# Order changes around a product scheme: second-layer operands, two plain projections, weight sums

## The reference

```
scores = scale * q @ k.T          # 4 x 8 heads of 576 x 64
ret    = scores * Dmat            # Dmat[i, j] = gamma_h ** (i - j) for i >= j, else 0
x      = (ret @ v), heads side by side                       # 2304 x 512
h      = x @ w_in                                            # 2304 x 2048
g      = h if h >= 1; 0 if h <= -1; (h + 1)**2 / 4 between   # the gate
x      = g @ w_out                                           # 2304 x 512
out    = ((x @ w_a) * (x @ w_b)) @ w_out2                    # 2304 x 1536, then 2304 x 512
```

## Time and profile before

| | |
|---|---|
| median of the runs | 897.81 us |
| profiled execution, its own time | 899.2 us |
| span in its profile | 897.4 us |
| PE busy | 864.2 us, 96% |
| DVE busy | 516.6 us, 58% |
| ACT busy | 349.0 us, 39% |
| POOL busy | 186.7 us, 21% |

### The profile page before, as it was taken

How to read it: one execution, slowest core, us unless ns; L and a number is a source line. 1 busy time by engine, 2 the same in 40 slices (tenths; PEclk the granted TensorE clock), 3 DMA queues, 4 the chain that set the end, 5 groups by cost and what they waited for, 6 DMA issues and landing times.

```text
span 897.4 us, 14103 instructions
## 1 busy us (share of the span) xinstructions
PE 864.2 (96%) x5520; PEld 825.6 (92%) x5520; DVE 516.6 (58%) x873; ACT 349.0 (39%) x650; POOL 186.7 (21%) x198
## 2 busy tenths in 40 slices
PE   7999999999999999999899888999999999999998
PEld 6989998999899999999899877889999999999996
DVE  4686777674545764446866555674434475434353
ACT  1235664554553443434433444342223242223220
POOL 4652125301422232323452233100000000000000
PEclk9999999999999999999999999999999999999999
DMA  9999179867453644463253744565454755454622
GB/s 354 322 367 360 45 248 379 334 218 294 173 184 125 249 176 168 173 237 139 106 203 161 280 190 159 215 235 211 165 211 164 247 199 211 165 211 164 209 73 70
DMA packets 47665, 188.35 MB, mean 210 GB/s; under 512 B 3568, under 2 KB 16368, under 8 KB 38896
## 3 DMA queue, kind: packets, MB, share of 16 engines
q1 hardware_dynamic: 47456, 187.26, 56.9%
q10 hardware_dynamic: 144, 0.20, 0.1%
HBM read 137.63 MB, written 49.81 MB: 209 GB/s over the span
## 4 chain that ended last, share of the span: by engine, by line
PE 80%; DVE 11%; ACT 4%; issue 2%; DMA 1%; SPq 1%; POOL 0%; ACTq 0%; DVEq 0%; POOLq 0%
PE score_b L684 7%; PE score_b L688 7%; PE score_b L686 7%; PE score_a L684 5%; PE score_a L688 5%; PE score_a L686 5%; PE kv_b L724 3%; PE kv_b L725 3%; PE kv_b L723 3%; PE ret_b L724 3%; PE ret_b L725 3%; PE ret_b L723 3%; PE ret_b L707 2%; PE ret_b L705 2%; PE kv_b L707 2%; PE kv_b L705 2%
## 5 line engine op out<-in xcount | busy, mean ns | idle before, releaser
L684 PE MATMUL score_b<-xop_hi,wop 128*128 128x384 f32 x416 | 140.3, 337 | 10.5 <-DVE wop L843 7.3
L688 PE MATMUL score_b<-xop_hi,wop 128*128 128x384 f32 x416 | 139.5, 335 | 0.0
L686 PE MATMUL score_b<-xop_lo,wop 128*128 128x384 f32 x416 | 139.3, 335 | 0.0
L684 PE MATMUL score_a<-xop_hi,wop 128*128 128x384 f32 x312 | 104.7, 336 | 9.1 <-DVE wop L843 6.0
L686 PE MATMUL score_a<-xop_lo,wop 128*128 128x384 f32 x312 | 104.2, 334 | 0.0
L688 PE MATMUL score_a<-xop_hi,wop 128*128 128x384 f32 x312 | 104.2, 334 | 0.0
L684 PEld LDWEIGHTS score_b<-xop_hi,wop 128*128 128x128 f32 x416 | 78.1, 188 | 14.8 <-issue 8.8
L686 PEld LDWEIGHTS score_b<-xop_lo,wop 128*128 128x128 f32 x416 | 78.1, 188 | 1.2
L688 PEld LDWEIGHTS score_b<-xop_hi,wop 128*128 128x128 f32 x416 | 78.1, 188 | 0.0
L1230 ACT ACTIVATE p<-score_b 128x384 f32<-128x384 f32 x52 | 25.5, 490 | 115.7 <-PE score_b L688 115.7
L684 PEld LDWEIGHTS score_a<-xop_hi,wop 128*128 128x128 f32 x312 | 58.6, 188 | 10.8 <-issue 10.2
(11 more groups left out here) (166 smaller groups left out, 2120.2 us busy)
## 6 DMA issues: line engine op xcount, KB each, us to landing
wop<-w_ops SPq DMA_DIRECT2D x40, 1792.0 KB, 7.3
w_ops<-wop SPq DMA_DIRECT2D x12, 1792.0 KB, 6.0
kq<-k_q SPq DMA_DIRECT2D x16, 576.0 KB, 6.8
wo_raw<-w_out SPq DMA_DIRECT2D x9, 1024.0 KB, 9.8
kvt<-kv_tok SPq DMA_DIRECT2D x16, 512.0 KB, 5.8
w_ops<-s_op SPq DMA_DIRECT2D x8, 1024.0 KB, 5.9
wo_hi<-w_outs SPq DMA_DIRECT2D x8, 1024.0 KB, 6.9
wo_lo<-w_outs SPq DMA_DIRECT2D x8, 1024.0 KB, 9.1
```

Source lines behind the costliest of these rows:

```text
L684: pe.matmul(o, w[:, 0, at], xop_hi[b][:, k, :], start=(start and k == 0), stop=False, skip_group_check=True)
L686: pe.matmul(o, w[:, 0, at], xop_lo[b][:, k, :], start=False, stop=False, skip_group_check=True)
L688: mm = pe.matmul(o, w[:, 1, at], xop_hi[b][:, k, :], start=False, stop=(k == 1), skip_group_check=True)
```

## The change

- **Second layer's operands.** The sums' half of step u + 1 is rounded and split in the middle of step u (before: at its end), and the raw half of step u + 2 at the end of step u (before: that of u + 1 in its middle). POOL does all four low parts of a step first, and then the sums of u + 2 instead of u + 1.
- **Last two projections.** `project(1, 14)` moves from ahead of the product steps into step 0, and `project(1, 15)` from step 0 into step 1, both before product 5. `copy_y` of tile 1 moves from step 1 to step 2.
- **Copies and gate.** In steps 0 to 2 ACT copies product 5 right after the third relu. The gate's four relus write prod0, prod1, prod0, prod1 instead of prod1, prod0, prod0, prod1; the first waits for DVE's gate and no longer for POOL.
- **Weights' sums.** The table of gates behind which the eight sets are rounded and split changes, and SP issues the load and the slabs of pair p + 2 ahead of the store of set p.

```diff
-        prep_steps = {(0, 10): 0, (0, 12): 1, (0, 14): 2, (1, 0): 3, (1, 2): 4, (1, 4): 5, (1, 6): 6,
+        prep_steps = {(0, 9): 0, (0, 12): 1, (1, 1): 2, (1, 2): 3, (1, 4): 4, (1, 5): 5, (1, 7): 6,
                       (1, 8): 7}
...
+            for p in range(2):
+                load_s(p)
+            for p in range(2):
+                store_slabs(p)
             for p in range(NF1 // 2):
-                load_s(p)
-                store_slabs(p)
-                if p:
-                    store_s(p - 1)
-            store_s(NF1 // 2 - 1)
+                if p + 2 < NF1 // 2:
+                    load_s(p + 2)
+                    store_slabs(p + 2)
+                store_s(p)
...
                 if v <= V1:
-                    low_parts(v - 1, 0)
-                    low_parts(v - 1, 1)
-                if 0 <= v + 1 - V1 < NF2:
-                    second_sums(v + 1 - V1)
-                if v <= V1:
-                    low_parts(v - 1, 2)
-                    low_parts(v - 1, 3)
+                    for i in range(4):
+                        low_parts(v - 1, i)
+                if 0 <= v + 2 - V1 < NF2:
+                    second_sums(v + 2 - V1)
...
-            project(NT - 1, NF1 - 2)
...
-                if v == 0:
-                    project(NT - 1, NF1 - 1)
-                else:
+                if v:
                     pe.wait_ge(u2_copied, v)
                     product(7, v - 1, main_b[(v - 1) % 2], False).then_inc(p7_done, 1)
+                if v < 2:
+                    project(NT - 1, NF1 - 2 + v)
...
-                s = [prod1, prod0, prod0, prod1][i]
+                s = [prod0, prod1, prod0, prod1][i]
...
-                if v == 1:
+                if v == 2:
                     copy_y(NT - 1)
                 if 0 <= u + 1 < NF2:
-                    split_ops(u + 1, 0)
+                    split_ops(u + 1, 1)
...
-                if 0 <= u + 1 < NF2:
-                    split_ops(u + 1, 1)
+                if 0 <= u + 2 < NF2:
+                    split_ops(u + 2, 0)
...
-                if p and i < 2:
+                if p and i == 0:
+                    act.wait_ge(g_ready, 4 * p - 1)
+                elif p and i == 1:
                     act.wait_ge(gl1_ready, 4 * p)
                 elif i >= 2:
-                    act.wait_ge(g_ready, 4 * p + 2)
-                    if i == 3:
-                        act.wait_ge(gl1_ready, 4 * p)
+                    act.wait_ge(g_ready, 4 * p + i - 1)
...
-                if 0 <= u + 1 < NF2:
-                    round_ops(u + 1, 0)
                 if gated_before:
                     gate_relu(v - 1, 2)
+                if v < 3:
+                    copy_p5(v)
+                if gated_before:
                     gate_high(v - 1, 2)
...
+                if 0 <= u + 1 < NF2:
+                    round_ops(u + 1, 1)
-                if v == 1:
+                if v == 2:
                     copy_y(NT - 1)
...
-                if v < V:
-                    if v:
-                        act.wait_ge(b1_ready, v)
-                    act.wait_ge(p5_done, v + 1)
-                    nc.scalar.activation(p5[:, :], p5_b, ACT.Copy).then_inc(p5_copied, 1)
+                if 3 <= v < V:
+                    copy_p5(v)
...
-                if 0 <= u + 1 < NF2:
-                    round_ops(u + 1, 1)
+                if 0 <= u + 2 < NF2:
+                    round_ops(u + 2, 0)
```

More of the change, by code:

```diff
@@ L1186, in gate_high, with copy_p5 @@
                                      ACT.Copy).then_inc(gh1_ready, 1)
+            def copy_p5(v):
+                if v:
+                    act.wait_ge(b1_ready, v)
+                act.wait_ge(p5_done, v + 1)
+                nc.scalar.activation(p5[:, :], p5_b, ACT.Copy).then_inc(p5_copied, 1)
             def step(v):
```

## The result

The changed kernel takes 890.82 us (median of 4 runs, 889.48 to 892.33), before 897.78 (4 runs). The ratio is 0.992, 95% interval 0.9908 to 0.9933. It is faster by 7.0 us, where 18.8 were forecast; 890.8 lies above the range of 874 to 886. The profiled execution took 892.33 us, span 890.5.

A forecast was written before the change was run, and what follows sets the result against it. PE bounds the kernel, its matmuls unchanged, so only its idle or slow time can shrink. Gains of 14.2 + 2.0 + 2.6 = 18.8 us gave 879.0 us; forecast 876 to 882, range 874 to 886.

The forecast's parts named there:

- Term 1: Second layer's steps: operands written half a step sooner remove PE's waits on wop, net gain 14.2 us (10.5 to 16.0).
- ten waits: PE's waits for DVE's wop write before the second layer's steps 0, 1, 4 to 11: 16.0 us, all to go.
- what comes back: Second layer's steps 3 and 4: other work limits them, so 0.9 us each, 1.8 us, of the gain is lost.
- The second rival: Second layer: DVE replaces wop as the bound, half of eight waits returns, time 886 us; chance 0.13.
- Term 2: Plain tiles and weights' sums: gain at the change of tiles less a tile 1 wait, net 2.0 us (-3 to 5.2).
- The gain at the change of tiles: Change of plain tiles: xl starts sooner and partly escapes POOL's sums, gaining 3.0 us (1.5 to 5.2).
- The first rival: Tile 1: the weights' sums become the wait, making term 2 -3 us and the time 884; chance 0.15.
- set 7: Tile 1: POOL's last set of the weights' sums was to begin at 175.5 and end at 179.5.
- the gap: Tile 1, ahead of the projection of f = 9: PE waits some 1.0 us for gl.
- The turn from a set to the next but one: Weights' sums in tile 1: 6.2 us of SP issues, 5.9 of landing and 4.3 of sums, 16.4 us.
- they now stand ahead of each store of sums: Tile 1: SP's load and four slab stores, 6.2 us, precede each store of sums and make the sums later.
- Term 3: First product steps: last two projections in steps 0 and 1 cover ACT and DVE, gaining 2.6 us (1.5 to 3.45).

The follow-up runs named there:

- 12: Changed kernel with fourth wop load first, slabs early, POOL waiting for xl, later y copies; plus sums' half split behind prod0 in steps 3, 4: 877.97 us.
- 11: Changed kernel with fourth wop load first, slabs early, POOL waiting for xl, later y copies; plus three POOL sums in each of steps 3, 4: 878.85 us.
- 8: Changed kernel with the fourth wop load first and the table of gates as before, SP's order still new: 882.62 us.
- 7: Changed kernel with the fourth wop load first and SP's order as before, the table of gates still new: 885.83 us.
- 6: Changed kernel with the fourth wop load first, all slabs stored during tile 0 and six sets of sums one gate sooner: 880.44 us.
- experiment 3: Changed kernel with the fourth product step's wop load issued ahead of the first two output weights' loads: 884.66 us.

## Why the prediction was wrong

**Term 1 held in its mechanism and was 1.2 us too large.** All ten waits went, as said. The term was 14.2 and is 13.0; what I mis-sized was what comes back. By PE's starts of product 1 the second layer's steps 3 and 4 took 17.8 us before (487.43 to the 505.25 of the earlier trace rows) and take 17.5 now:

```profile
487.43 0.33 PE L684 MATMUL score_b<-xop_hi,wop 128*128 128x384 f32 x1
```

```profile
491.28 0.33 PE L682 MATMUL score_b<-xop_hi,wop 128*128 128x384 f32 x1
...
499.22 0.45 PE L682 MATMUL score_a<-xop_hi,wop 128*128 128x384 f32 x1
...
508.74 0.44 PE L682 MATMUL score_b<-xop_hi,wop 128*128 128x384 f32 x1
```

Waits of 2.9 us have gone from them and they are only 0.4 us shorter, so 2.5 us came back there instead of 1.8. Another 1.5 came back in step 0, where I had put nothing: the wait of 1.05 us ahead of step 1 went, but PE now waits 1.2 us for b in the step, which got 0.5 us longer. The later steps gave 1.0 us more than their waits. What step 4 of the changed kernel spends its time on can be read from ACT and DVE:

```profile
505.40 0.53 ACT L1226 ACTIVATE ph<-prod 128x384 fp32r<-128x384 f32 x1 [1.87 <-DVE prod L978]
505.83 1.04 ACT L1063 ACTIVATE wop<-wop_sum 128x1024 fp32r<-128x1024 f32 x1
```

```profile
506.91 1.31 DVE L841 TENSOR_TENSOR wop<-wop_sum,wop 128x1024 fp32r<-128x1024 f32 x1 [1.60 <-ACT wop L1063]
508.14 0.55 DVE L992 TENSOR_TENSOR prod<-score_b,a 128x384 f32<-128x384 f32 x1
```

ACT rounds prod1's product (505.40) and then the sums' half (505.83); DVE waits 1.60 us for this, splits it (506.91), and only then multiplies prod0 (508.14). Prod0 ends at 508.69, and product 1 of step 5, which needs it, starts at 508.74. So the two engines take turns, and I had summed each engine's work, not the turns. This chain is read from the trace. Taking the split out of it (12) shortened the two steps by only 0.5 us, because product 1 needs the split too; so that the turns and no other limit set these steps is argued, not shown. POOL's part in it is small (11). The second rival was right in kind for these two steps, but not for the long ones.

**Term 2: the gain was larger and the loss much larger.** The gain at the change of tiles is 4.3 us (3.0 forecast). The first rival came: POOL's set 7 began 3.4 us later than estimated, and I had given the gap 1.0 us. It was 4.25 us (4.4 from matmul to matmul), and I had no price for what follows a gap of that length: nearly 5 us of matmuls at the lower level of 1.2 GHz, which lost 2.3 us more. PE was also 0.5 us later than before when it came to the change of tiles, for which no part of the change accounts. 4.3 - 4.4 - 2.3 - 0.5 is the net of -2.7 that the marks show, to within 0.2. The rival's -3 had that size, and I gave it 0.15. The turn from a set to the next but one, 16.4 us in the estimate, was 17.4 and 18.6, with landings of 7.2 to 8.2 us where I took 5.9; and my own sum for set 7 slipped by 0.5 us, since 159.6 + 16.4 is 176.0 and not 175.5. The step as I put it ("they now stand ahead of each store of sums") blamed SP's order, which is nearly free (8); the new table of gates makes the chain late (7), and slabs stored in tile 1 seem to keep it late (6, where gates and slabs were moved together).

**Term 3 failed, and it took the forecast out of its range.** The step was "the last two projections ... stand in steps 0 and 1 and cover what ACT and DVE do there". They did, and saved 4.2 us by the marks, or 2.8 by experiment 3, where 2.6 were forecast. But I asked only ACT and DVE who is helped by the later end of a projection, not SP, which waits for exactly that end ahead of the output weights' loads; and behind these in one queue stands the load that step 3 needs. The wait and the low clock after it, 7.6 us by the marks, are the largest part of the 11.9 us missing; with one load moved ahead in SP's order (3) 6.2 of them came back, to 884.66 us, inside the range. Had I priced only this and kept the rest, the forecast would have been 886.6, and with the measured term 2 in its place 891.3; the errors of term 1 and of what term 3 saves nearly cancel.

## What to carry to other kernels

When work is moved on the engine that sets the time, list everyone who waits for its end, DMA queues too, and what stands behind them in those queues: a transfer that landed 4.4 us ahead of its use lost that, and 4.8 us more, to 4 MB issued a moment earlier. Each of the two gaps of over 4 us on PE cost another 2.3 or 2.5 us of low clock, so the two together were worth 14. In a ring of two buffers, where each set waits for the store two sets back, moving one early set moved all the later ones, here with the DMA engines full behind it. Where two engines hand a step's pieces to each other, follow the turns as well as the busy time of each, and see what the next product waits for once one turn is gone.

## What the runs showed of the hardware

- The granted clock fell to 0.50 after gaps of 4.25 and 4.78 us and came back about 5 us after PE had started again (186.42 to 191.1, 237.09 to 242.3); the gaps of 1.4 us ahead of the second layer's steps 4 and 5 in the kernel before left it at 1.00 (496 to 518 us).
- Four DVE subtractions of 128x384 with both inputs in SBUF took 4.11 us beside POOL's sums and 1.96 without them. The Trainium skill (SBUF — State Buffer, "Who interferes with whom") says that a DVE instruction with two SBUF inputs contends with a GpSimd instruction that reads SBUF, and this trace agrees. What it costs depends on who waits: six more POOL sums in steps 3 and 4 cost 0.7 us together (11).
- A wop load of 1.8 MB landed 14.7 us after its issue with 4 MB issued in the 2 us ahead of it, 9.5 us with the last of the 4 MB issued 7 us ahead (before), and 7.3 us when it was issued ahead of them (3). That it is what is issued ahead of it that counts was shown (3); whether only in the same queue was not tried.
